# Attention in a fused kernel: the global columns of two heads side by side, one transpose for both

## The reference

```python
scores = scale * (q @ k^T)                      # per head, 768 x 768
keep   = (key < n_global) | (0 <= row - key < n_local)    # n_global 8, n_local 96
bias   = -slope[head] * (n_local if key is only global else row - key)
a      = softmax(where(keep, scores + bias, -1e9))
x      = a @ v                                  # (1536, 512) after the heads are put side by side
x      = (h * tanh(softplus(h))) @ w_out,  h = x @ w_in
out    = sum over 4 experts of share_e * relu(x @ w1_e) @ w2_e
```

## Time and profile before

| | us |
|---|---|
| median of 3 runs | 903.66 (902.88 to 904.01) |
| the profiled execution | 902.35 |
| its span, first to last instruction | 900.5 |
| TensorE busy in the span | 873.6 (97%) |
| VectorE busy | 483.3 (54%) |
| ScalarE busy | 319.2 (35%) |
| GpSimd busy | 257.6 (29%) |
| attention, start of the span to its last output | about 150 |

### The profile page before, as it was taken

How to read it: one execution, slowest core, us unless ns; L and a number is a source line. 1 busy time by engine, 2 the same in 40 slices (tenths; PEclk the granted TensorE clock), 3 DMA queues, 4 the chain that set the end, 5 groups by cost and what they waited for, 6 DMA issues and landing times.

```text
span 900.5 us, 12637 instructions
## 1 busy us (share of the span) xinstructions
PE 873.6 (97%) x4916; PEld 444.9 (49%) x4916; DVE 483.3 (54%) x1010; ACT 319.2 (35%) x597; POOL 257.6 (29%) x218
## 2 busy tenths in 40 slices
PE   6888999999999999999999999999999999999998
PEld 6666876444444444444444444444444444444443
DVE  7756887999999989874542125222134322212121
ACT  4898886545555656552021110102010111101020
POOL 1278993222222222210029200077000292000000
PEclk9987999999999999999999999999999999999999
DMA  9871420000000000202000500001300000000001
GB/s 214 276 237 37 142 84 1 1 1 1 1 7 3 1 1 1 97 1 94 10 1 0 186 1 1 6 0 53 134 1 6 0 0 0 1 24 23 35 12 49
DMA packets 52004, 39.19 MB, mean 44 GB/s; under 512 B 40816, under 2 KB 41712, under 8 KB 51440
## 3 DMA queue, kind: packets, MB, share of 16 engines
q1 hardware_dynamic: 49888, 34.31, 12.5%
q10 hardware_dynamic: 2064, 4.19, 1.3%
HBM read 35.35 MB, written 3.15 MB: 43 GB/s over the span
## 4 chain that ended last, share of the span: by engine, by line
PE 89%; ACT 5%; DVE 4%; issue 1%; POOL 0%; DVEq 0%
PE bank L607 67%; PE bank L676 14%; PE bank L546 2%; PE bank L578 2%; ACT scaled L865 2%; PE bank L597 2%; ACT tmp L849 1%; ACT tmp L890 1%; PE bank L501 1%; DVE xT L1213 1%; PE bank L559 1%; DVE tmp L1117 1%; ACT hid L839 0%; DVE tmp L1228 0%; DVE tmp L1346 0%
## 5 line engine op out<-in xcount | busy, mean ns | idle before, releaser
L961 ACT ACTIVATE hid<-bank 128x512 f16<-128x512 f32 x96 | 57.3, 597 | 422.2 <-PE bank L607 422.2
L607 PE MATMUL bank<-xT,wA 128*128 128x512 f16 (+1 forms) x864 | 194.6, 379 | 0.0
L1337 DVE SCALAR_TENSOR_TENSOR hid<-bank,hid 128x512 f16<-128x512 f32 x96 | 66.4, 691 | 181.8 <-ACT hid L961 181.8
L607 PEld LDWEIGHTS bank<-xT,wA 128*128 128x128 f16 x864 | 84.5, 98 | 100.6
L676 PE MATMUL bank<-hid,wB 128*128 128x512 f16 x576 | 132.2, 379 | 0.9 <-DVE xT L1213 0.9
L607 PE MATMUL bank<-xT,wB 128*128 x576 | 125.3, 379 | 0.0
L607 PE MATMUL bank<-wA,hid 128*128 128x512 f16 x576 | 125.3, 379 | 0.0
L607 PE MATMUL bank<-wB,hid 128*128 128x512 f16 x576 | 125.3, 379 | 0.0
L815 POOL TENSOR_TENSOR tmp<-tmp 128x512 f32<-128x512 f32 x48 | 61.4, 1280 | 190.2 <-DVE tmp L1360 190.2
L770 POOL TENSOR_SCALAR stage<-stage,sc 128x1024 f32<-128x1024 f32 x32 | 36.0, 1124 | 256.7 <-DVEq L1330 250.4
L1417 DVE SCALAR_TENSOR_TENSOR acc<-bank,pg,acc 128x512 f32<-128x512 f32 x36 | 27.0, 750 | 131.7 <-PE bank L607 131.7
(11 more groups left out here) (111 smaller groups left out, 948.8 us busy)
## 6 DMA issues: line engine op xcount, KB each, us to landing
stage<-in_moe_w SPq DMA_DIRECT2D x8, 2048.0 KB, 9.8
stage<-in_moe_w_in SPq DMA_DIRECT2D x1, 4096.0 KB, 16.6
wB<-in_moe_w_out ACTq DMA_DIRECT2D x1, 4096.0 KB, 16.3
hid<-in_q SPq DMA_DIRECT2D x16, 192.0 KB, 3.4
hid<-in_k SPq DMA_DIRECT2D x16, 192.0 KB, 3.5
xT<-in_v SPq DMA_DIRECT2D x8, 384.0 KB, 5.0
out_y<-acc SPq DMA_DIRECT2D x12, 256.0 KB, 2.0
rows<-max SPq DMA_DIRECT2D x4, 128.0 KB, 4.1
```

What stands on the lines that cost most here:

```text
L607: last = pe.matmul(dst, lhs(c, a), rhs(c, b), start=(c == 0 and n == 0), stop=(c == chunks - 1 and n == 2))
L961: act.activation(hv[:, f, 0, :], psum(f % 4), ACT.Relu).then_inc(f_hi, 1)
L1337: dve.scalar_tensor_tensor(hv[:, f, 1, :], psum(f % 4), 0.0, hv[:, f, 0, :], ALU.max, ALU.subtract).then_inc(f_ready, 1)
```

## The change

The two exponentials of a far query tile's two heads are put in one buffer of 576 columns, head 0's with its global columns last, head 1's with its global columns first, so that the 2 x 32 global columns lie side by side. They share one transpose of 64 columns, done with head 1's unit: 2 transposes for an even far unit, 3 for an odd one. The transposed block has head 0's global keys on partitions 0 to 31 and head 1's on 32 to 63. P*V of either head contracts the local blocks as before and the shared block over those 64 partitions, against a new small copy of V (`vg`) that is zero on the other head's 32 partitions. Around it:

- SyncE loads V's first 32 keys a second time, twice 64 KB (`vg_all`), behind q and k of pair 1 and before V of pair 1. GpSimd clears `vg`, sets its columns of ones, waits for these loads, and splits them in halves (`split_second_heads`), pair 0 before its second all-reduce, pairs 1 to 7 behind it.
- ScalarE copies the distance table for the odd far units (32 + 256 columns) before it splits V of pair 0.
- Three memsets of 96 columns (L1043) go.
- Even units need their neighbour's evictions before P*V, so P*V stands three units behind (`PV_LAG`), `pT_b` has four buffers, and the output steps move by one. In the last pair P*V of units 8 and 9 both stand in step 11, before the piece of the next stage.
- The wider matmul of a score comes first in both orders of columns.

```diff
@@ -66,6 +66,20 @@
     BAND_COLS = sum(BAND_W[:3])
+    W = BAND_W[2]
+    def far(u):
+        return u // 2 >= 2
+    def unit_blocks(u):
+        blks = band[u // 2]
+        return blks[-1:] + blks[:-1] if far(u) and u % 2 else blks
+    def table_at(u):
+        return BAND_COLS if far(u) and u % 2 else BAND_AT[u // 2]
@@ -165,6 +179,10 @@
         kT_sb = [scratch(S) for _ in range(2)]
+        FIRST, SECOND = slice(0, GLOBAL_COLS), slice(GLOBAL_COLS, 2 * GLOBAL_COLS)
+        BOTH = slice(0, 2 * GLOBAL_COLS)
+        vg_all = scratch(PAIRS * D)[BOTH].rearrange("p (m d) -> p m d", d=D)
+        vg = scratch(2 * PAIRS * VD)[BOTH].bitcast(F16).rearrange("p (s a m d) -> p s a m d", s=2, a=2, d=VD)
@@ -173,14 +191,13 @@
-        W = 3 * P
-        dist_b, key_b = (scratch(BAND_COLS) for _ in range(2))
-        s_b = [scratch(W) for _ in range(3)]
-        pT_b = [scratch(W).bitcast(F16).rearrange("p (s n) -> p s n", s=2) for _ in range(3)]
+        dist_b, key_b = scratch(BAND_COLS + W), scratch(BAND_COLS)
+        s_two = [scratch(2 * W) for _ in range(2)]
+        pT_b = [scratch((2 + n % 2) * P).bitcast(F16).rearrange("p (s n) -> p s n", s=2) for n in range(4)]
...
-        rel_b = dist_b
+        rel_b = dist_b[:, 0:BAND_COLS]
...
@@ -342,6 +361,7 @@
         FILL_AT = [0, 2, 4, 6]
+        PV_LAG = 3
@@ -366,12 +386,21 @@
+        def unit_cols(u, banded):
+            return offsets(unit_blocks(u) if banded else full[u // 2])[1]
+        def s_b(u):
+            at = W * (u % 2)
+            return s_two[u // 2 % 2][:, at:at + unit_cols(u, True)]
...
                 return bank[2][:, 0:S], pT_g
-            n = len(band[u // 2]) * P
-            return psum(4 + u % 2, n), pT_b[u % 3][:, :, 0:n]
+            n = P * ((2 + u % 2) if far(u) else len(band[u // 2]))
+            return psum(4 + u % 2, n), pT_b[u % 4][:, :, 0:n]
@@ -424,6 +453,8 @@
                     load_pair(0, 1)
+                    for a, rows_a in enumerate((FIRST, SECOND)):
+                        sp.dma_start(vg_all[rows_a], v_d[0:GLOBAL_COLS, a * QT::2 * QT]).then_inc(vg_loaded, 16)
@@ -511,7 +542,7 @@
-                blks = (band if banded else full)[u // 2]
+                blks = unit_blocks(u) if banded else full[u // 2]
@@ -529,6 +560,7 @@
                 head = slice(a * D, (a + 1) * D)
+                runs.sort(key=lambda run: -run[1])
@@ -568,34 +600,50 @@
                 pe.wait_ge(p_ready, PB * i + UNITS * slot + u + 1)
-                src = s_b[u % 3] if banded else s_g
                 dst, _ = p_out(u, banded)
                 at = UNITS * (2 * i + slot) + u
                 if banded and at >= 2:
                     pe.wait_ge(pT_act, at - 1)
                     pe.wait_ge(pT_dve, at - 1)
-                for b in range(len((band if banded else full)[u // 2])):
-                    last = pe.transpose(dst[:, b * P:(b + 1) * P], src[:, b * P:(b + 1) * P], ident[:])
+                if banded and far(u):
+                    two = s_two[u // 2 % 2]
+                    start = W + GLOBAL_COLS if u % 2 else 0
+                    for b in range(2):
+                        last = pe.transpose(dst[:, b * P:(b + 1) * P], two[:, start + b * P:start + (b + 1) * P], ident[:])
+                    if u % 2:
+                        last = pe.transpose(dst[0:2 * GLOBAL_COLS, 2 * P:3 * P],
+                                            two[:, W - GLOBAL_COLS:W + GLOBAL_COLS], ident[:])
+                else:
+                    src = s_b(u) if banded else s_g
+                    for b in range(len((band if banded else full)[u // 2])):
+                        last = pe.transpose(dst[:, b * P:(b + 1) * P], src[:, b * P:(b + 1) * P], ident[:])
                 last.then_inc(pT_psum, 1)
             def pv(i, slot, u, banded):
                 m = 2 * i + slot
                 qt, a = u // 2, u % 2
-                pe.wait_ge(pT_act, UNITS * m + u + 1)
-                pe.wait_ge(pT_dve, UNITS * m + u + 1)
+                shared = banded and far(u)
+                needs = u + 1 - u % 2 if shared else u
+                pe.wait_ge(pT_act, UNITS * m + needs + 1)
+                pe.wait_ge(pT_dve, UNITS * m + needs + 1)
                 if u == 0:
                     pe.wait_ge(v_split, m + 1)
+                if shared and u == 4 and m < 2:
+                    pe.wait_ge(vg_split, m + 1)
                 if u in (0, UNITS // 2):
                     pe.wait_ge(o_ready, 2 * m + 1 + u // (UNITS // 2))
                 _, pt = p_out(u, banded)
-                keys = [kt for kt, _ in (band if banded else full)[qt]]
+                keys = [(kt, b) for b, (kt, n) in enumerate((band if banded else full)[qt]) if n == P]
                 dst = psum(6 + u // (UNITS // 2), VD, (u % (UNITS // 2)) * VD)
-                for b, kt in enumerate(keys):
+                parts = [(pt[:, :, b * P:(b + 1) * P], v_parts(m)[:, :, a, kt]) for kt, b in keys]
+                if shared:
+                    parts.append((pT_b[(u + 1 - a) % 4][BOTH, :, 2 * P:3 * P], vg[:, :, a, m]))
+                for b, (p_b, v_b) in enumerate(parts):
                     for n, (x, y) in enumerate(((0, 0), (0, 1), (1, 0))):
-                        last = pe.matmul(dst, pt[:, x, b * P:(b + 1) * P], v_parts(m)[:, y, a, kt],
-                                         start=(b == 0 and n == 0), stop=(b == len(keys) - 1 and n == 2))
+                        last = pe.matmul(dst, p_b[:, x], v_b[:, y],
+                                         start=(b == 0 and n == 0), stop=(b == len(parts) - 1 and n == 2))
                 last.then_inc(pv_done, 1)
             def split_product(dst, lhs, rhs, chunks, fresh=None, only=None):
@@ -624,9 +672,13 @@
                     if banded:
-                        ahead, behind = reach(i, slot, u, 3), reach(i, slot, u, -2)
+                        ahead, behind = reach(i, slot, u, 3), reach(i, slot, u, -PV_LAG)
...
                             scores_of_two(*ahead)
+                        if not after(i, slot) and u == UNITS - 1:
+                            pv(*behind, banded)
+                            pv(i, slot, UNITS - 3, banded)
+                            behind = None
@@ -783,8 +835,33 @@
+            def split_second_heads(n, pairs):
+                pool.wait_ge(v_scale, n + 1)
+                src = vg_all[:, pairs]
+                pool.tensor_scalar(src, src, scale_cols(v_col(n))[2][BOTH], 1.0, ALU.mult, ALU.mult).then_inc(vg_part, 1)
+                pool.wait_ge(vg_part, 5 * n + 1)
+                for a, rows_a in enumerate((FIRST, SECOND)):
+                    src, hi, lo = vg_all[rows_a, pairs], vg[rows_a, 0, a, pairs, 0:D], vg[rows_a, 1, a, pairs, 0:D]
+                    pool.tensor_scalar(hi, src, 1.0, 1.0, ALU.mult, ALU.mult).then_inc(vg_part, 1)
+                    pool.wait_ge(vg_part, 5 * n + 2 * a + 2)
+                    pool.tensor_tensor(lo, src, hi, ALU.subtract).then_inc(vg_part, 1)
+                    pool.wait_ge(vg_part, 5 * n + 2 * a + 3)
+                pool.sem_inc(vg_split, 1)
+            pool.wait_ge(iotas, 3)
+            pool.memset(vg, 0.0).then_inc(vg_ones, 1)
+            pool.wait_ge(vg_ones, 1)
+            for a, rows_a in enumerate((FIRST, SECOND)):
+                pool.memset(vg[rows_a, 0, a, :, D:VD], 1.0).then_inc(vg_ones, 1)
+                pool.wait_ge(vg_ones, 2 + a)
+            pool.wait_ge(vg_loaded, 32)
...
                 col = v_col(n)
+                if n == 2:
+                    split_second_heads(1, slice(1, PAIRS))
+                if n == 1:
+                    split_second_heads(0, slice(0, 1))
...
@@ -877,6 +953,10 @@
                     expo(0, 0, 1, banded)
+                    near = BAND_COLS - GLOBAL_COLS
+                    act.copy(dist_b[:, BAND_COLS:BAND_COLS + GLOBAL_COLS], dist_b[:, near:BAND_COLS])
+                    act.copy(dist_b[:, BAND_COLS + GLOBAL_COLS:BAND_COLS + W],
+                             dist_b[:, near - 2 * P:near]).then_inc(second_table, 1)
@@ -1038,10 +1118,7 @@
             dve.wait_ge(iotas, 3)
-            dve.scalar_tensor_tensor(rel_b, rel_b, -1.0e9, rel_b, ALU.mult, ALU.max)
-            for s in s_b:
-                last = dve.memset(s[:, 2 * P + GLOBAL_COLS:3 * P], 0.0)
-            link(last)
+            link(dve.scalar_tensor_tensor(rel_b, rel_b, -1.0e9, rel_b, ALU.mult, ALU.max))
...
@@ -1110,12 +1187,14 @@
                 m = 2 * i + slot
-                width = offsets((band if banded else full)[qt])[1]
                 if banded:
+                    width = unit_cols(u, banded)
+                    if m == 0 and u == 5:
+                        dve.wait_ge(second_table, 1)
...
                     dve.sem_inc(carrier, 1)
-                    dve.tensor_tensor_reduce(s_b[u % 3][:, 0:width], psum(u % 3, width),
-                                             dist_b[:, BAND_AT[qt]:BAND_AT[qt] + width],
+                    dve.tensor_tensor_reduce(s_b(u), psum(u % 3, width),
```

(16 more changed lines are left out.)

## The result

The changed kernel took 916.33 us (median of 4 runs, 916.03 to 916.79) beside 903.27 for the kernel before (4 runs, 902.48 to 904.01): a ratio of 1.0145 (95% interval 1.013 to 1.016), 13.1 us slower. The forecast was 6.5 us slower, 910.2 us with a range of 900.5 to 918. The direction was right and the time lies in the range, but the loss is twice what I had added up, and the time is outside the forecast's own range of 906 to 914. The profiled execution took 916.03 us, its span is 914.1.

A forecast was written before the change was run, and what follows sets the result against it. TensorE was taken to bound attention from the last half of pair 3 through pair 7, ScalarE or start-up waits mostly elsewhere. Terms -3.0 + 8.3 + 0.7 + 0.5 = +6.5 us gave 910.2 us, range 900.5 to 918.

The forecast's parts named there:

- P*V three behind: P*V one unit later in TensorE's queue: same work issued, waits for evictions no longer than before, 0.
- Transposes removed: 32 fewer TensorE transposes in far units, 0.11 us each, 3.5 us in all, struck in pair 0: -3.0 us.
- Change of row count: 64-row P*V stalls weight loads 0.23 us a far unit: 47 units less idle time +8.3 us, pair 3 +0.7.
- Half clock doubles a stall: Pair 3, thin cover under ScalarE: three units at 3 x 0.23 x 2 = 1.4 us, half shown, +0.7 us.
- Shared transpose: The transpose of 64 columns in odd far units: no stall of its own, 0.
- rival 2: Shared transpose changes the mode as well, or a change costs 0.17 us: 915 to 920 us, chance 0.15.
- The start: Two small loads delay the first all-reduce and V of pair 1; GpSimd's work falls in idle time: +0.5 us.
- Rival 1: A lone 64-row P*V matmul does not stall, only paired scores do: 901.2 us, faster, chance 0.17.
- Rival 3: The stalls hide in idle time and ScalarE's exponentials, along with the saving: 903.7 to 905 us, chance 0.06.
- Rival 4: Stalls of pairs 4 to 6 let TensorE's clock fall, 5 us lost each time: 915 to 925 us, chance 0.05.

The follow-up runs named there:

- the version with both edits: Changed kernel with VectorE instead of GpSimd splitting pair 0's global keys of V, and the shared block contracted over 128 rows: 905.94 us, ratio 1.0013.
- the slice of rows: Kernel before, with only its three P*V matmuls over the global block contracting over rows 0 to 63 instead of 128: 915.17 us, ratio 1.014.
- the filler: Changed kernel with 16 unread identity products in TensorE's step 9 of pair 0, before the late scores: 911.96 us, ratio 1.0084.
- best version: As the version with both edits, with small loads behind V of pair 2, VectorE's split in step 4, 8 unread products in step 9: 900.28 us, ratio 0.9964.
- the moved output step: The best version with VectorE's last output step of the previous pair in step 5 instead of 4: 901.81 us, ratio 0.9968.

## Why the prediction was right in direction and half the size

The mechanism that carries the forecast, a stall at each change of row count, was found and priced right. The sum was 6.6 us short: 2.5 by the row count, 3.3 by P*V three behind, 0.4 by the start and 0.3 by the transposes. That 916.3 us still lies in the range owes something to luck: the room above 914 was there for a dearer change of row count and for a fallen clock in pairs 4 to 6, and neither happened.

- **Transposes removed, -3.0 us: about right.** By the medians, the version with restored row count is 1.5 us above before (0.17% of 904.6); take off the lag (3.3) and GpSimd (0.9), and -2.7 us is left for the transposes and the narrower copies; it is a remainder and was not measured alone.
- **Change of row count, +8.3 and +0.7 us: mechanism and unit price right, total measured 11.5.** 0.11 in and 0.12 out are the forecast's 0.10 and 0.13. What was off is the conversion to time. I counted 47 units at full price and 17 at nothing, with 0.5 us of idle time taking some of it in a pair. Changed kernel less the version with restored rows gives by pair -1.0, +3.2, +2.6, +0.2, +1.0, +0.9, +0.9 and +1.5 us. In pairs 4 to 6 the eight stalls, 1.84 us, cost half of that, so more of them is absorbed than I took; in pairs 1 and 2, which I had called "nearly as before", they cost 5.8 us. In pair 1 the clock goes with it (0.75 for 0.88); in pair 2 it is nearly the same (0.82 for 0.83), and what makes its 2.6 us is not shown.
- **Half clock doubles a stall, my term for pair 3: wrong.** At the turn from pair 0 to pair 1 both kernels below are at the lower level of the clock. First the changed kernel, then the version with both edits, whose rows are restored, both from the chain:

```profile
37.11 0.73 PE bank L645 x9
37.84 0.40 PE bank L619
38.24 0.61 PE bank L645 x9
```

```profile
36.63 0.61 PE bank L645 x9
37.24 0.27 PE bank L619
37.50 0.49 PE bank L645 x9
```

  The differences are 0.12, 0.13 and 0.12 us, as at full clock. The stall is a time, not a number of TensorE's cycles.
- **Shared transpose, 0: right**, and with it the second half of rival 2 is out; its first half, 0.17 us a change, fell with the measured 0.11 and 0.12. The Trainium skill (TensorEngine Tiling (Array Packing), Restrictions and Gotchas) excludes column tiling of fp32 transposes; the 0.11 us of L614 agrees.
- **P*V three behind, 0: the step that failed most.** The forecast followed the wait for the neighbour's eviction and asked nothing of the output steps, which move by one with it. Measured 3.3 us, half of what was missing. Asking of each step tied to the same offset what is queued behind it would have found the part in the full-clock pairs (0.4 us each): a 0.55 us multiplication moved in front of masked scores in VectorE's queue. The other 2 us, in pairs 0 to 3, have no shown cause.
- **The start, +0.5: size near, the larger reason missed.** I sized the loads, and the first all-reduce is 0.46 us later. "Fall where it is busy for 0.55 of 21.3 us" took GpSimd's idle time for free time. The row that gives it away stands in the trace of the kernel before, where the first ordinary instruction behind the all-reduces has 11.30 us of idle time that nothing ends:

```profile
27.85 0.36 POOL L790 PARTITION_ALL_REDUCE sc<-sc  x1 [14.46 <-DVE sc L1203]
39.51 0.90 POOL L795 TENSOR_SCALAR xT<-xT,sc 128x768 f32<-128x768 f32 x1 [11.30 <-issue]
```

  Alone this costs 0.9 us (median, 0.1 to 1.7 by its interval), in the changed kernel it lengthens TensorE's wait from 1.42 to 3.21 us.
- **The rivals.** Rival 1 (a lone 64-row matmul does not stall) fell with the chain of pair 5 and with the slice of rows alone, +1.4%. The Trainium skill (TensorE: Matmul & The Clock Gate, closing table of "Why this matters for your kernels") gives a matmul over few rows the time of a full one. For the matmul itself the trace agrees (in pair 5 of the changed kernel 194 ns over 64 rows, 195 over 128), but it leaves out the change. The Trainium skill (TensorEngine Tiling (Array Packing), Key Properties) has the drain at a change of mode, and the trace agrees with it, at 0.23 us for in and out together. Rival 3 (the stalls hide) fell with the same runs. Rival 4 had the right cause in the wrong place: pairs 4 to 6, where I looked for a fallen clock, kept 1.00, and it fell in pairs 0 and 1 (0.77 for 0.92, 0.75 for 1.00) and in pair 3 (0.68 for 0.74).

The parts, as measured one at a time, sum to -2.7 + 11.5 + 3.3 + 0.9 = 13.0 us for the 13.1, but this closes in part by construction, since -2.7 is what the others leave. They do not simply add either: undoing GpSimd's part gave nothing while the stalls were in, and the filler gave 5.5 us with them in. In pairs 4 to 6, where the clock is out of play, they do: before 14.4, lag +0.4, rows +0.9, and -0.7 from the lag's version to that with the shared transpose and restored rows (14.8 to 14.1) make the 15.0 of the changed kernel. These steps, too, are differences of one row of versions and must close; the check from outside is the slice of rows put into the kernel before, 0.8 us in pair 5 for the 0.9 here.

**Open.** What tips the clock was not settled. The wait of 1.42 us before the late scores left it up in the trace of the kernel before and in no other without a filler, with stalls or without. The best version had 0.91 in pair 3 and the one with the moved output step 0.77. Single executions of the kernel with the slice of rows went from 911.8 to 923.3 us, so part of every figure here that runs through the clock is a mean over such cases. The lag alone was not tried with a filler, so how much of its 3.3 us is the clock's is not known. The small loads were never moved by themselves.

## What to carry to other kernels

Leave the number of contracted rows alone inside a stream of small matmuls: fill the block up to 128 rows with zeros, since 64 rows saved nothing and two changes cost 0.23 us. When a step moves by one place in an engine's queue, look at every other step tied to the same offset, and at what is queued behind it; here that was 0.4 us in each pair at full clock, and 3.3 us in all came with the longer lag, for an "unchanged" amount of work. Price idle time of TensorE in a partly busy stretch by what the granted clock does in the stretch behind it, not by its own length, and on GpSimd look for idle time that nothing ends before calling it free.

## What the runs showed of the hardware that I had not expected

- GpSimd: 8.44 us of idle time from an all-reduce to the first ordinary instruction in the changed kernel, 8.27 us to one that is a single column wide, and 6.02 and 7.79 us before the next all-reduce, all with no releaser in the profile. Of the last two, 1.83 and 1.37 us lie behind the arrival of its input.
- TensorE's stall at a change of row count has the same length, 0.11 to 0.13 us, at both levels of the clock.
- With these stalls TensorE stays at the lower level for longer: 17.1 us with them and 6.9 without behind the same wait of 1.42 us (GpSimd's split taken out, and both edits, one trace each).
- A transpose of a 64-column fp32 block right behind transposes of 128 columns has no stall: 0.11 us each.
- The clock can be bought: 16 unread products before one wait kept pair 1 at 1.00 (14.6 us for 18.4), and with 8 the best version stands at a ratio of 0.9964, without them at 0.999.
